# Splitting the second weight matrix inside the first middle step of a fused attention, mixing and gating kernel

## The reference, cut to what matters

```python
out = sm_attn(pool4(q), pool4(k), pool4(v))  # pooled by 4, then repeated 4 times
    + banded_attn(q, k, v)                   # |i - j| < 4
x  = out as (tokens, features)
u  = x + real(fft(fft(x, axis=tokens), axis=features))
un = (u - mean(u)) / sqrt(var(u) + 1e-6)
x2 = u + maximum(un @ w_ch1, 0) @ w_ch2      # 512 -> 2048 -> 512
gate = sigmoid(causal_conv5(x2))             # per feature
y  = (gate * (x2 @ w_val)) @ w_out
```

## Time and profile before

| | us |
|---|---|
| median of 3 runs | 855.63 (854.61 to 857.05) |
| the profiled execution | 854.21 |
| its span | 852.4 |
| PE busy | 739.1 (87%) |
| DVE busy | 437.0 (51%) |
| ACT busy | 204.5 (24%) |
| GpSimd busy | 61.2 (7%) |
| opening, to the first `mlp_up` | 167.2 |

### The profile page before, as it was taken

One profiled execution on the slowest core, in us unless ns is written; L12 is line 12 of the kernel. 1 busy time (PEld: TensorE's weight loads), 2 busy tenths in 40 slices (PEclk: granted clock), 3 DMA queues, 4 the chain that ended last, 5 costly groups with the idle time before them and its releaser, 6 DMA issues.

```text
span 852.4 us, 15400 instructions
## 1 busy us (share of the span) xinstructions
PE 739.1 (87%) x5956; PEld 547.4 (64%) x5956; DVE 437.0 (51%) x955; ACT 204.5 (24%) x409; POOL 61.2 (7%) x80
## 2 busy tenths in 40 slices
PE   1843554689989999899999999899999999999998
PEld 1721222457767677678767667677676777777776
DVE  7832466975445358464354477554263483112542
ACT  1211358512221111222221212122221122111101
POOL 2000021300011021000010020000110120000000
PEclk9999995589999999999999999999999999999999
DMA  9813323260130010441220001711300000000001
GB/s 289 242 47 92 90 71 126 56 152 16 40 83 4 1 57 29 142 77 32 49 49 2 29 29 47 180 26 31 82 13 1 1 28 29 1 2 1 1 12 45
DMA packets 58746, 49.05 MB, mean 58 GB/s; under 512 B 27504, under 2 KB 52208, under 8 KB 57584
## 3 DMA queue, kind: packets, MB, share of 16 engines
q1 hardware_dynamic: 50032, 31.59, 15.0%
q10 hardware_dynamic: 8640, 16.43, 5.6%
HBM read 43.29 MB, written 4.72 MB: 56 GB/s over the span
## 4 chain that ended last, share of the span: by engine, by line
PE 63%; SPq 15%; DVE 9%; issue 5%; DMA 5%; ACT 2%; POOL 1%; DVEq 0%; ACTq 0%; POOLq 0%
PE P L465 19%; PE Y L481 17%; SPq L349 10%; PE P L588 4%; PE Y L588 4%; PE Y L577 4%; PE A L490 3%; SPq L343 3%; DMA kl<-qk_win 2%; SPq L345 2%; PE A L436 2%; PE A L380 2%; PE A L538 1%; PE A L532 1%; DMA vl<-v_win 1%
## 5 line engine op out<-in xcount | busy, mean ns | idle before, releaser
L465 PE MATMUL P<-unT,w 128*128 128x288 f16 x1536 | 215.6, 292 | 8.1 <-issue 4.6
L481 PE MATMUL Y<-hT,w 128*128 128x288 f16 x1536 | 214.9, 286 | 1.5 <-DVE xT L1034 1.5
L1013 DVE SCALAR_TENSOR_TENSOR hT<-P,hT 128x288 f16<-128x288 f32 x128 | 58.4, 457 | 262.2 <-ACT hT L694 262.2
L465 PEld LDWEIGHTS P<-unT,w 128*128 128x128 f16 x1536 | 150.7, 100 | 54.9 <-issue 12.0
L481 PEld LDWEIGHTS Y<-hT,w 128*128 128x128 f16 x1536 | 144.9, 98 | 45.5 <-issue 7.0
L694 ACT ACTIVATE hT<-P 128x288 f16<-128x288 f32 x128 | 52.6, 411 | 198.4 <-PE P L465 198.4
L1049 DVE SCALAR_TENSOR_TENSOR gate<-xT,cw,gate 128x288 f32<-128x288 f32 x128 | 66.4, 519 | 4.5
L665 ACT ACTIVATE prob_or_un<-prob_or_un 73x288 f32<-73x288 f32 (+1 forms) x52 | 23.3, 448 | 171.8 <-DVE prob_or_un L884 171.8
L384 PE MATMUL Y<-mask_sb,idb_sb 128*128 128x304 bf16 x5 | 2.2, 431 | 35.4 <-DMA kl<-qk_win 35.4
L588 PE MATMUL P<-shared,wo 128*128 128x288 f32 x128 | 32.1, 409 | 0.7 <-DVE shared L1061 0.5
L588 PE MATMUL Y<-shared,wo 128*128 128x288 f32 x128 | 32.1, 409 | 0.5 <-DVE shared L1061 0.5
(11 more groups left out here) (141 smaller groups left out, 863.0 us busy)
## 6 DMA issues: line engine op xcount, KB each, us to landing
w<-w_ch ACTq DMA_DIRECT2D x8, 1024.0 KB, 8.7
vl<-v_win SPq DMA_DIRECT2D x80, 76.0 KB
kl<-qk_win SPq DMA_DIRECT2D x40, 140.0 KB, 3.7
ql<-qk_win SPq DMA_DIRECT2D x20, 256.0 KB, 5.1
pair_or_folded<-qk_pool SPq DMA_DIRECT2D x8, 580.0 KB, 5.0
pair_or_spectrum<-qk_pool SPq DMA_DIRECT2D x8, 580.0 KB, 5.5
out<-ot ACTq DMA_DIRECT2D x32, 144.0 KB, 1.8
x<-v_pool SPq DMA_DIRECT2D x4, 576.0 KB
```

The lines of the kernel that those rows point to most:

```text
L465: last = mm(P[s % 2][:, 0:HN], w1s[:, k, f * 128:(f + 1) * 128, wt], unT[:, ut, k, ha * HN:(ha + 1) * HN], start=k == 0 and wt + ut == 0, ...
L481: last = mm(Y[d][:, 0:HN], w2s[:, f, d * 128:(d + 1) * 128, wt], hT[s % 3][:, ht, :], start=f == 0 and wt + ht == 0, stop=f == KF - 1 and ...
L1013: nc.vector.scalar_tensor_tensor(out=hT[s % 3][:, 1, :], in0=P[s % 2][:, 0:HN], scalar=0.0, in1=hT[s % 3][:, 0, :], op0=ALU.max, op1=ALU.s ...
```

## The change

The first middle step, `step(1, 0)`, is written out ahead of the loop on PE, ACT and DVE, and the loop runs from 1. SP's and GpSimd's loops stay as they were. Where the code asked `isinstance(b, int)` to tell the opening from the loop, it now asks `opening(b)`, so the written-out step uses the banks and waits of a middle step.

Only chunks 8 and 9 are begun in the opening. The rest is done in slots 0 to 7 of the written-out step: ACT runs `weights(10 + s)` behind `relu(s)` in slots 0 to 7 (six of them with a high, all eight with an in-place copy), DVE runs `weight_low(9 + s)` behind `hidden_low(s)` in slots 1 to 6. PE waits for the chunk that it is about to read, and `conv(m, 0, 0)` on DVE, the first writer of `gate`, for all 16.

```diff
+def opening(b):
+    return isinstance(b, int) and b == 0
...
                 if part == 0:
                     pe.wait_ge(hid_sb, n + 1)
                     if s == 0:
-                        pe.wait_ge(w_split, 2 * WCH)
                         pe.wait_ge(step_over, b + 1)
+                    if opening(b) and s < KF:
+                        pe.wait_ge(w_split, WCH + s // 2 + 1)
...
-            with pe.Fori(0, B - 1) as it:
+            step(1, 0)
+            with pe.Fori(1, B - 1) as it:
...
                         relu(m, s)
+                        if opening(m) and s < WCH:
+                            weights(WCH + 2 + s)
...
-                    for c in range(WCH, WCH + 4):
+                    for c in range(WCH, WCH + 2):
                         weights(c)
                     for g in range(5):
                         spectrum(b, g)
                     for j in range(3):
-                        weights(WCH + 4 + j)
                         odd_part(b, j)
                     for i in range(6):
                         u_columns(b, i, m)
-                        if i == 1:
-                            weights(WCH + 7)
                         un_columns(b, i)
-                    for c in range(WCH + 8, 2 * WCH + 2):
-                        weights(c)
...
+                        elif opening(b) and d == 0:
+                            dve.wait_ge(w_split, 2 * WCH)
...
                         hidden_low(m, s)
+                        if opening(m) and 1 <= s < WCH - 1:
+                            weight_low(WCH + 1 + s)
...
-                    for c in range(WCH, WCH + 5):
+                    for c in range(WCH, WCH + 2):
                         weight_low(c)
                     combine(b, 0)
-                    weight_low(WCH + 5)
...
                     columns(b, 1)
-                    weight_low(WCH + 6)
...
                     for i in range(2, 6):
                         columns(b, i)
-                    weight_low(WCH + 7)
```

More of the change, by code:

```diff
@@ L236, in banks @@
         def banks(b, u):
-            if isinstance(b, int):
+            if opening(b):
                 return Y[u % 2], Y[2 + u % 2], P[u % 2]
@@ L249, in mixed_banks @@
         def mixed_banks(b, j):
-            return (Y[0:2], Y[2:4], A)[j] if isinstance(b, int) else A
+            return (Y[0:2], Y[2:4], A)[j] if opening(b) else A
         def add_mixed(add, tile, r, upper, lower):
@@ L260, in column_banks @@
         def column_banks(b, i):
-            return (Y[2 * i % 4], Y[(2 * i + 1) % 4]) if isinstance(b, int) else (A[i % 2], A[i % 2])
+            return (Y[2 * i % 4], Y[(2 * i + 1) % 4]) if opening(b) else (A[i % 2], A[i % 2])
         def tokens(tile):
@@ L366, in unit_scores @@
                 n = b * NU + u
-                read = n - 1 if isinstance(b, int) else n
+                read = n - 1 if opening(b) else n
                 if later(read):
@@ L398, in unit_transpose @@
                     pe.wait_ge(scaled, NT * b + u - UD + 1)
-                if not isinstance(b, int):
+                if not opening(b):
                     if u == 0:
@@ L421, in unit_av @@
                 n = b * NU + u
-                if u < UD or not isinstance(b, int):
+                if u < UD or not opening(b):
                     pe.wait_ge(probT_done, n + 1)
-                if isinstance(b, int) and u >= 2:
+                if opening(b) and u >= 2:
                     if u < UD + 2:
@@ L523, in mix_feat @@
                     pe.wait_ge(spec_sb, 5 * b + 5)
-                elif not isinstance(b, int):
+                elif not opening(b):
                     pe.wait_ge(em_done, 3 * b + j)
@@ L700, in spectrum @@
                         act.wait_ge(mixed_o, 3 * b)
-                    bank = [A[0], A[1], P[0], P[1], Y[3]][g] if isinstance(b, int) else A[g % 2]
+                    bank = [A[0], A[1], P[0], P[1], Y[3]][g] if opening(b) else A[g % 2]
                     nc.scalar.copy(sp_sb[0:m, g, :], bank[0:m, 0:HS]).then_inc(spec_sb, 1)
@@ L848, in _ @@
             step(0, None)
-            with act.Fori(0, B - 1) as it:
+            step(1, 0)
+            with act.Fori(1, B - 1) as it:
                 step(it + 1, it)
@@ L1174, in _ @@
             dve.wait_ge(ld_const, CONSTS)
-            with dve.Fori(0, B - 1) as it:
+            step(1, 0)
+            with dve.Fori(1, B - 1) as it:
                 step(it + 1, it)
```

## The result

| | before | changed |
|---|---|---|
| median of 19 executions each | 854.36 (853.29 to 858.38) | 856.45 (853.21 to 862.02) |
| the profiled execution | 854.21 | 856.17 |
| its span | 852.4 | 854.2 |
| PE busy | 739.1 | 742.9 |

The ratio is 1.0033, 95% interval 1.0016 to 1.0049: some 2 us slower, where 6.5 us less were forecast.

What follows compares the result with a forecast made beforehand. PE was taken to bound the kernel after the opening's chain of waits. 854.2 - 6.8 + 2.7 - 2.4 = 847.7, 6.5 less; from the runs' median of 855.6 that gave 849.1 us, range 845.3 to 852.4.

Steps and rivals of the forecast that it cites:

- Steps (1) to (4): Opening: chunks 10, 11 gain 4.8, chunk 13's low 1.7, chunk 14's low 0.6, v load gives back 0.3; sum 6.8 us.
- The second rival: Later part of the opening was hidden anyway, gain there only 4.8 us: 851.1 us in all; chance 0.12.
- Steps (5) and (6): First middle step: DVE's lows cost 1.96 us in slots 1 to 3 and 0.7 in slots 4 to 6; sum 2.7.
- The fifth rival: First middle step: ACT and DVE fall into step within one slot, six slots cost 15 us: 861.4; chance 0.05.
- a sign of being wrong: First middle step: the prediction is wrong if the slots up to 7 lose more than 5 us.
- Step (7): Written-out border: PE no longer stands still at the jump, gain 2.4 us, bounds 0 and 4.0.
- the fourth rival: Low bound of DVE's cost, and the clock held at the border: 10.2 us less, 845.4; chance 0.12.
- The third rival: PE's 2.3 us at a step's border stay, at the loop's entry or within written-out code: 851.5; chance 0.18.
- the loop now jumps back once instead of twice: Borders: of PE's two stops at jumps, 2.36 and 2.25 us, one row of about 2.3 us should remain.
- The gain survives until the end: From slot 7 on, PE and the window loads its products release set the pace and move along, keeping the gain.
- the limit for `mlp_up(2)`: Written-out border: `relu(0)` can't precede issue of the last output's DMA, 358.2, so third `mlp_up` starts at 359.15, not 361.53.
- The branch price: Skill's 51 ns per branch, 108 ns per compare-and-branch: one jump less worth 0.2 us, whole change 4.3.

Runs made afterwards that it cites:

- run 4: The changed kernel with all three middle steps written out on PE, ACT and DVE, no loop there: 851.33 us, ratio 0.9964.
- run 8: The changed kernel with 32 empty instructions and the chunks' work moved to later slots of the first middle step: 847.13 us, ratio 0.9926.
- run 2: The changed kernel with 32 empty semaphore instructions at the start of PE's program: 850.31 us, ratio 0.9958.
- run 1: The kernel before with the middle step written out as in the change, all 16 chunks still split in the opening: 858.11 us, ratio 1.0048.
- run 5: Control: the kernel before with 32 empty instructions at the start of PE's program: 854.70 us, ratio 1.0007.
- run 7: The changed kernel with 8 empty instructions at the start of PE's program: 857.57 us, ratio 1.0044.
- run 3: The kernel before with 224 empty instructions at the start of PE's program: 888.72 us, ratio 1.0395.
- run 11: Run 8 with the load of v's second half released by GpSimd after PE's last projection, not by ACT's step end: 844.49 us, ratio 0.9882.
- run 9: Run 8 without the 32 empty instructions: 852.59 us, ratio 0.9972.
- run 6: Run 1 with 32 empty instructions at the start of PE's program: 853.93 us, ratio 0.9994.
- run 10: Run 8's late chunks with all three middle steps written out, no loop on PE, ACT and DVE: 844.83 us, ratio 0.9889.
- run 12: Runs 10 and 11 together, late chunks, no jumps and the v load released early: 843.06 us, ratio 0.9860.

## Why the prediction was wrong

**Steps (1) to (4), the opening: right in the trace of the change.** `spectrum` 4.90 earlier (4.8 forecast), `combine(1)` 6.68 (6.5), `normalise(2)` 7.24 (7.1), `hidden_low(0)` 7.1 (6.8). The load took 5.4 us again, so the 0.3 that I gave back were not lost. The second rival is out. In the traces of the other kernels with the short opening the gain at `hidden_low(0)` is 5.1 (run 4) to 7.7 us (run 8), so one execution does not fix it to a tenth.

**Steps (5) and (6): near in sum, partly by luck.** 7.1 in slot 2 becomes 3.9 in slot 7: 3.2 lost, 2.7 forecast. The product's wait is 1.74, not 2.5, 1.15 longer than before. What made up for it stands in no term: behind the first matmuls PE runs at half clock for 5.6 us, from 169.0 to 174.6, where before it was 2.7, from 176.2 to 178.9. The 2.9 us more at half clock are some 1.4 us lost. Slots 5 and 6 lose the 0.7. The fifth rival is out. But the longer wait has a price beyond its length, which I had not counted: run 2 lost 2.7 us more in this step, behind a wait of 2.35 us for that product, at the 1.2 GHz level from 183.0 to 189.1. With 5.9 us lost up to slot 7, that trace passes the 5 us that the prediction named as a sign of being wrong. Run 8, whose chunks stand later, loses nothing in it.

**Step (7), the border that is written out: right.** From -4.3 to -7.9, 3.6 in place of 2.4, within the bound of 4.0: the clock came too, as the fourth rival had it (3.10 us for 24 matmuls, not 4.78). The third rival is out: the loop's entry costs PE nothing.

Two steps failed, beside 1.3 us in the starting point (855.6 from three executions, 854.36 from 19). By slot 2 of the second step the change had gained 7.9 us, more than the forecast, and at the end it was 1.8 behind.

**The first failed step is the sum's silent one: that the jump that is left costs what it cost.** I took "the loop now jumps back once instead of twice" as the whole effect on the border and never asked where the jump's target now lies. Writing out a step moved the body. PE stops again 16 entries behind the target, and the two stops together with the longer half clock cost 3.3 us more at this border, in the changed kernel and in run 1. Runs 2, 5 and 7 show that it is the place: 32 empty instructions take the stop away, 8 leave it and bring it nearer to the jump by 8 entries, and in the kernel before, where the first stop alone was there, 32 cost nothing. Run 3 puts it into the kernel before.

**The second is "The gain survives until the end".** It cost more in this trace than the first. In the second step the changed kernel lost 2.9 us and 2.8 more, in two places. The first is E: pooled v's second half is loaded when ACT has sent off the last output, and 3.6 us that PE comes earlier are not matched by ACT. DVE waits 1.23 us for it, PE 1.90 instead of 0.59, and then the granted clock falls from 365.8 to 369.2. In run 8 a wait of 1.61 us at this place, without a fall, costs 1.0 us; in run 11 wait and loss are gone. I had put that very chain down as the limit for `mlp_up(2)`, and did not ask what else `step_over` releases. The second is a wait of 1.98 us for a window load at 429.32, 1.20 in the kernel before, with half clock from 430.6 to 434.1. I did not test it by itself, and it stays open. In run 8, where PE comes 11 us earlier than before, the same wait is 1.21, so arriving earlier doesn't suffice to make it.

One more thing stays open here. From slot 2 to its end the second step loses 5.7, 3.6, 4.0 and 5.8 us in the four kernels with the second stop in their loop (the change, runs 1, 7 and 9), 1.3, 2.8 and 1.0 in those with 32 empty instructions (runs 2, 6 and 8), though the stop comes only behind this step. The medians don't settle it: the 32 give back 6.1, 4.2 and 5.5 us (6.4, 4.6 and 3.9 by the ratios), and in the traces the border alone is 3.1, 4.9 and 5.3 us cheaper with them. Whether the code's place acts in the second step too, or the clock fell there by chance, no run separates.

Run 2, the changed kernel without its second stop, is at 850.31, 3.8 under its kernel before. Its trace is 3.5 under: 7.1 from the opening, 5.5 lost in the first step where 2.7 were forecast, 3.7 from the border, 1.3 lost in the second step, 0.5 behind it. Run 8, with the chunks placed later, is 7.5 under.

The branch price of the Trainium skill ("Advanced Engine Details and Errata", section Control Flow Timing), which I weighed in the prediction, is not what a jump back costs PE. Taken, it left PE idle for 2.23 to 2.93 us in all eleven traces that have one. PE's own record of the compare-and-branch lasts 6.4 to 7.2 us where the branch is taken (in the changed kernel the matmuls issued before it cover the first 4.4), and 0.083 where it isn't. DVE's record lasts 0.063 taken and 0.055 not taken in the kernel before.

What PE waits for at these stops has no releaser in the timeline, but the traces' DMA packets show it. Beside the loads, the DMA engines carry packets of a kind named instruction. Run 4, which has no jump on PE, has 47 of them on queue q8:

```profile
q8 instruction: 47, 0.77, 0.4%
```

Each is 16,384 bytes long, and PE passes 254.8 entries from one to the next on average (255.1 and 255.0 in runs 10 and 12): they bring PE's program, block by block. In straight code they come in time. At the remaining border of the changed kernel one starts at 535.51, takes 0.92 us, and PE's first matmul behind the jump is at 538.03. The next starts only at 538.62, takes 0.96 us, and PE goes on at 540.81. In run 2 the next one starts at 536.75 and PE doesn't stop, since by the count below it still has 240 entries of the first block to run. At all 14 taken jumps and all 6 second stops PE goes on 1.2 to 1.8 us after such a packet has ended. So both stops are waits for instructions, and the second comes when the jump lands shortly before the end of a block.

The places fit fixed blocks. The second stop keeps its place in the order of what PE runs while the loop's body moves under it: 16 and 8 entries behind the jump. With one pass of the loop (3094 entries) taken off per jump, it stands ahead of entry 4289 of the program in the changed kernel and of 1473 in run 3, 2816 apart, which is 11 times 256. Blocks of 64 are out: run 5's jump lands 204 entries ahead of 1473, so that one of them would end 12 entries behind the target, and it has no second stop. The other engines' loops agree: DVE's body has 381 entries, and its first entry behind a taken jump comes 2.7 to 3.0 us after the branch, while ACT's (245), SP's (153) and GpSimd's (35) come after 0.17 to 0.25. Other stops of PE without a releaser, in the opening's straight code, moved along with the empty instructions, so they are of another kind.

"Advanced Engine Details and Errata", section ISA Cache, in the Trainium skill, states cache lines of 256 instructions. The traces agree: 16,384 bytes for some 255 entries.

## What to carry to other kernels

A change to the length of straight code ahead of a loop moves the loop's body: before judging the change, run it again with a few dozen empty instructions in front. When a border or a stage gets shorter, list everything that the slow engine at its end releases, loads above all, and not only the first waiter. And count a new wait of 1.5 to 2 us on PE, where PE bounds the kernel, as possibly more than its length (the falls below): keep added work out of the slots where another engine's chain is the one that PE waits for.

## What the hardware showed that I had not expected

- 32 instructions that do nothing make a kernel of 856 us 6 us faster (856.45 against 850.31), and 224 of them, 0.151 us apart, delay PE's first matmul by 29.5 us.
- A second stop 8 to 16 entries behind a jump's target costs 1.74 to 2.30 us of idle time, and 3.3 to 3.8 at a border with the clock behind it.
- The trace's DMA packets of kind instruction show when each block of PE's program was fetched, and so which stop without a releaser is a wait for code.
- In PE's full stretches the granted clock fell behind some waits and not behind others, and the length of the wait doesn't decide it: within run 1 it fell behind 1.47 us at 369.08 and not behind 2.23 us at 433.54; it fell behind 1.90 at 364.83 in the changed kernel and not behind 1.61 at 360.30 in run 8. The falls cost 1.5 to 3 us each. With one trace for each kernel I can't tell what decides it, nor how much of the wider spread of the changed kernel (9 us against 5) comes from it.
